# Weight splits ahead of the scatters, and the first expert block on two turns' rows

## The reference, cut to what matters

```python
def _moe_ref(x, w_gate, w_noise, noise, w1, w2):
    ...
    noisy_logits = logits + noise_scale * noise
    top2 = np.argpartition(-noisy_logits, 2, axis=1)[:, :2]
    ...
    for e in range(E):
        for k in range(2):
            mask = top2[:, k] == e
            h = np.maximum(x[mask] @ w1[e], 0.0)
            out[mask] += top2_w[mask, k, None] * (h @ w2[e])

def reference(**kwargs):
    attn_out = _attn_ref(...)            # 4 batches, 8 heads, 576 tokens, head size 64; pool = 8
    x = attn_out as (2304, 512)
    x = _moe_ref(x, ...)                 # E = 8, w1 (8, 512, 1024), w2 (8, 1024, 512)
    return _moe2_ref(x, ...)             # max(0.01 h, h) with h = x @ w_in (512, 2048), then @ w_out
```

## Time and profile before

| | |
|---|---|
| median of three runs | 1105.24 us |
| profiled execution | 1103.91 us |
| its span | 1102.2 us |
| PE busy | 1033.5 us (94%) |
| DVE busy | 378.9 us (34%) |
| POOL busy | 379.6 us (34%) |
| mean granted TensorE clock | 0.967 of 2.4 GHz |

### The profile page before, as it was taken

The page is one execution under the profiler, slowest core; times in us unless marked ns, Lnnn a source line. Parts: engine busy times, 40 slices in busy tenths (PEclk is TensorE's granted clock), DMA queues, the critical chain, the costliest instruction groups (busy, mean ns, idle before and its releaser), DMA issues.

```text
span 1102.2 us, 16369 instructions
## 1 busy us (share of the span) xinstructions
PE 1033.5 (94%) x5180; PEld 870.6 (79%) x5181; DVE 378.9 (34%) x678; ACT 272.5 (25%) x497; POOL 379.6 (34%) x413
## 2 busy tenths in 40 slices
PE   5988289999999999999999995899999999999998
PEld 4887268888888888888888884788888888888887
DVE  5988542122212221222122212653333333333222
ACT  3443012222222222222222220232222222222222
POOL 3338691280917355371908202950100100000000
PEclk9988589999999999999999997899999999999999
DMA  8945452151524333251514212421101101001000
GB/s 296 337 145 189 178 160 77 57 180 39 171 67 140 97 111 127 80 158 49 173 63 144 95 38 72 147 78 39 39 20 58 39 20 58 20 1 39 1 1 38
DMA packets 53779, 105.75 MB, mean 96 GB/s; under 512 B 7408, under 2 KB 7536, under 8 KB 53744
## 3 DMA queue, kind: packets, MB, share of 16 engines
q1 hardware_dynamic: 35312, 63.33, 18.1%
q10 hardware_dynamic: 12672, 23.07, 6.3%
q0 software_dynamic: 5760, 18.88, 5.1%
HBM read 77.47 MB, written 27.79 MB: 95 GB/s over the span
## 4 chain that ended last, share of the span: by engine, by line
PE 79%; issue 9%; DVE 7%; POOL 3%; DMA 1%; ACT 1%; SPq 0%; POOLq 0%; DVEq 0%; ACTq 0%
PE ps L603 23%; PE ps L605 23%; PE ps L604 23%; PE ps L629 3%; POOL w_split L467 2%; PE ps L561 2%; PE ps L610 1%; PE ps L539 1%; POOL w_split L465 1%; PE ps L671 1%; DVE maxima L906 1%; PE ps L549 1%; DVE x L1149 1%; DVE k_sum L892 1%; DMA k_raw<-in_kT_dram 1%
## 5 line engine op out<-in xcount | busy, mean ns | idle before, releaser
L467 POOL TENSOR_TENSOR w_split<-w_raw,w_split 128x512 fp32r<-128x512 f32 x144 | 186.3, 1294 | 12.0
L465 POOL TENSOR_SCALAR w_split<-w_raw 128x512 fp32r<-128x512 f32 x144 | 92.3, 641 | 226.7 <-PE ps L605 224.7
L603 PE MATMUL ps<-w_split,xs_hi 128*128 (+1 forms) x344 | 138.4, 402 | 3.9 <-DVE xs_lo L1108 3.9
L603 PE MATMUL ps<-w_split,hT_hi 128*128 (+1 forms) x344 | 139.0, 404 | 2.0 <-DVE hT_lo L1115 2.0
L605 PE MATMUL ps<-w_split,hT_lo 128*128 (+1 forms) x344 | 135.4, 394 | 0.0
L605 PE MATMUL ps<-w_split,xs_lo 128*128 (+1 forms) x344 | 134.7, 391 | 0.0
L604 PE MATMUL ps<-w_split,hT_hi 128*128 (+1 forms) x344 | 134.6, 391 | 0.0
L604 PE MATMUL ps<-w_split,xs_hi 128*128 (+1 forms) x344 | 134.6, 391 | 0.0
L492 POOL DMA_INDIRECT y_in<-y_blocks,y_rows x36 | 34.8, 968 | 269.1 <-DVE x L1149 194.8
L603 PE MATMUL ps<-x_hi,w_split 128*128 128x512 f32 (+1 forms) x320 | 120.5, 377 | 1.4 <-DVE x_lo L1157 1.4
L604 PE MATMUL ps<-x_lo,w_split 128*128 128x512 f32 (+1 forms) x320 | 118.8, 371 | 0.0
(11 more groups left out here) (147 smaller groups left out, 1505.3 us busy)
## 6 DMA issues: line engine op xcount, KB each, us to landing
w_raw<-in_wall_dram SPq DMA_DIRECT2D x160, 256.0 KB
xs<-x_sorted ACTq DMA_DIRECT2D x45, 256.0 KB, 2.7
y_blocks<-y_sb ACTq DMA_DIRECT2D x43, 256.0 KB, 2.0
k_raw<-in_kT_dram SPq DMA_DIRECT2D x16, 288.0 KB, 5.5
q_sb<-in_qT_dram SPq DMA_DIRECT2D x18, 256.0 KB, 5.2
v_raw<-in_vT_dram SPq DMA_DIRECT2D x16, 288.0 KB, 5.2
out_dram<-h_sb SPq DMA_DIRECT2D x10, 256.0 KB, 2.0
x_sorted<-zero_rows SPq DMA_DIRECT2D x9, 256.0 KB, 4.1
```

The costliest lines, as they stand in the source:

```text
L465: pool.tensor_scalar(hi, w_raw[:, a, :], 1.0, 0.0, ALU.mult, ALU.add).then_inc(split_hi, 1)
L467: pool.tensor_tensor(lo, w_raw[:, a, :], hi.bitcast(F32), ALU.subtract).then_inc(split, 1)
L603: pe.matmul(out_ap, lhs_hi, rhs_hi, start=first, stop=False)
```

## The change

- POOL does all 16 splits of expert 0 first, then the 36 scatters, turn by turn.
- SP's queue gets a new order: the nine zero writes stand later, in groups of four and five, chunks 8 to 15 earlier. SP waits for the scatters of turns 0 and 1 and tells ACT by `x_landed` = 1, then for the rest, and tells it by `x_landed` = 2.
- DVE writes `first_needs` after turn 1: 1 if expert 0 already has 128 rows or more, else 2. ACT reads it into a register and loads block 0 when `x_landed` has reached it.
- DVE does `split_rows(0)` before the lists, and `list_y_rows` after `split_h(1)` and no longer after `split_rows(0)`.
- PE takes block 0 whole before `up(1)`, with `turn_rows(1)` between the two halves of `down(0)`. Only after that it waits for the lists. ACT loads block 1 after `copy_h(0)`.
- Scratch tables of the lists move from `q_sb` to `probsT` and `probs`, out of the way of the block tiles.

```diff
@@ SP
-            sp.wait_ge(zeros_made, 1)
-            for row in ZEROED:
-                sp.dma_start(x_sorted[row:row + P, :], zero_rows[:, :]).then_inc(x_zeroed, 16)
             load_w(4)
...
             load_w(8)
+            load_v(13)
+            load_w(9)
             load_q(13)
-            load_v(13)
+            load_w(10)
             load_v(14)
-            load_w(9)
+            load_w(11)
+            sp.wait_ge(zeros_made, 1)
+            for row in ZEROED[0:4]:
+                sp.dma_start(x_sorted[row:row + P, :], zero_rows[:, :]).then_inc(x_zeroed, 16)
             load_q(14)
+            load_w(12)
             load_v(15)
-            load_w(10)
+            load_w(13)
+            for row in ZEROED[4:]:
+                sp.dma_start(x_sorted[row:row + P, :], zero_rows[:, :]).then_inc(x_zeroed, 16)
+            load_w(14)
+            load_w(15)
             load_q(15)
-            load_w(11)
             load_q(16)
             load_q(17)
-            for n in range(12, CHUNKS):
+            for n in range(CHUNKS, CHUNKS + RING):
                 load_w(n)
+            sp.wait_ge(x_sent_early, 16 * EARLY_SENT)
+            sp.sem_inc(x_landed, 1)
+            sp.wait_ge(x_sent_late, 16 * (2 * TILES - EARLY_SENT))
+            sp.sem_inc(x_landed, 1)
+            for n in range(CHUNKS + RING, 2 * CHUNKS):
+                load_w(n)
@@ POOL
-            for n in range(SPLIT_FIRST):
+            for n in range(CHUNKS):
                 split_chunk(n)
-            n = SPLIT_FIRST
             for turn in range(len(TURNS)):
-                rows = rows_of(turn)
-                for at in range(0, len(rows), 2):
-                    send_rows(turn, rows[at:at + 2])
-                    if n < CHUNKS:
-                        split_chunk(n)
-                        n += 1
+                send_rows(turn, rows_of(turn))
@@ PE
                 for k in range(KF):
+                    if first and k == KF // 2:
+                        turn_rows(b + 1)
                     if k % 4 == 0:
                         pe.wait_ge(hT_split, b * 2 + k // 4 + 1)
...
-            pe.wait_ge(lists_ready, 1)
             turn_rows(0)
             up(0, 0)
-            turn_rows(1)
             turn_h(0)
+            down(0, 0, True)
+            pe.wait_ge(lists_ready, 1)
             up(1, expert_of(1))
             turn_rows(2)
-            down(0, 0, True)
             turn_h(1)
@@ ACT
-            act.wait_ge(x_sent, 16 * 2 * TILES)
+            act.wait_ge(first_known, 1)
+            needed = act.value_load(first_needs[0:1, 0:1], min_val=1, max_val=2)
+            act.wait_ge(x_landed, needed)
             act.dma_start(xs[:, :], x_sorted[0:P, :]).then_inc(xs_in, 16)
+            copy_rows(0)
+            relu(0)
+            copy_h(0)
             act.wait_ge(lists_ready, 1)
-            copy_rows(0)
+            act.wait_ge(x_landed, 2)
             load_rows(1)
-            relu(0)
             copy_rows(1)
             load_rows(2)
-            copy_h(0)
@@ DVE
+                    if PLACE_AT.index(step) == EARLY_TURNS - 1:
+                        dve.tensor_scalar(first_needs[:, :], row_of[0:1, 0:1], float(P), 1.0, ALU.is_lt,
+                                          ALU.add).then_inc(first_known, 1)
...
+            split_rows(0)
             n_e, nb, end, start, val, last_row, first_moved, moved = (e8[:, j, :] for j in range(8))
...
-            split_rows(0)
+            split_h(0)
+            split_rows(1)
+            copy_y(0, True)
+            split_rows(2)
+            split_h(1)
             list_y_rows()
-            split_rows(1)
-            split_h(0)
-            split_rows(2)
-            copy_y(0, True)
-            split_h(1)
```

More of the change, by code:

```diff
@@ L52 @@
 ROWS = DUMMY + P
+EARLY_TURNS = 2
+EARLY_SENT = 2 * TURN_FROM[EARLY_TURNS]
 BLOCKS = (2 * TOKENS + EXPERTS * (P - 1)) // P
@@ L97, in build @@
         block_end = sb("block_end", [1, EXPERTS], I32)
-        sb("to_64_bytes", [1, EXPERTS])
+        first_needs = sb("first_needs", [1, 1], I32)
         sb("to_2048_bytes", [P, 120])
@@ L240, in build @@
         y_listed = sem("y_listed")
-        x_sent = sem("x_sent")
+        x_sent_early = sem("x_sent_early")
+        x_sent_late = sem("x_sent_late")
+        x_landed = sem("x_landed")
+        first_known = sem("first_known")
         x_zeroed = sem("x_zeroed")
@@ L361, in _ @@
             load_w(8)
+            load_v(13)
+            load_w(9)
             load_q(13)
-            load_v(13)
+            load_w(10)
             load_v(14)
-            load_w(9)
+            load_w(11)
+            sp.wait_ge(zeros_made, 1)
+            for row in ZEROED[0:4]:
+                sp.dma_start(x_sorted[row:row + P, :], zero_rows[:, :]).then_inc(x_zeroed, 16)
             load_q(14)
+            load_w(12)
             load_v(15)
-            load_w(10)
+            load_w(13)
[3 more added lines that the diff above has]
+            load_w(15)
             load_q(15)
-            load_w(11)
             load_q(16)
             load_q(17)
-            for n in range(12, CHUNKS):
+            for n in range(CHUNKS, CHUNKS + RING):
                 load_w(n)
-            with sp.Fori(1, STAGES) as s:
+            sp.wait_ge(x_sent_early, 16 * EARLY_SENT)
[4 more added lines that the diff above has]
+                load_w(n)
+            with sp.Fori(2, STAGES) as s:
                 for c in range(CHUNKS):
@@ L426, in send_rows @@
                         out_offset=bass.IndirectOffsetOnAxis(ap=slots_i[:, tile, k:k + 1], axis=0),
-                        in_=x_rows[:, tile, :], in_offset=None).then_inc(x_sent, 16)
+                        in_=x_rows[:, tile, :], in_offset=None).then_inc(
+                            x_sent_early if turn < EARLY_TURNS else x_sent_late, 16)
             def rows_of(turn):
@@ L472, in await_last_use @@
                 pool.wait_ge(blocks_done, end)
-            pool.wait_ge(x_sent, 16 * 2 * TILES)
+            pool.wait_ge(x_sent_early, 16 * EARLY_SENT)
+            pool.wait_ge(x_sent_late, 16 * (2 * TILES - EARLY_SENT))
             for c in range(CHUNKS):
@@ L1044, in _, with split_rows, split_h, copy_y @@
             then = link
+            def split_rows(b):
+                dve.wait_ge(xs_hi_made, b + 1)
+                dve.tensor_tensor(xs_lo[:, :, :].rearrange("p a b -> p (a b)"), ps[:, XT_BANK, :],
+                                  xs_hi[:, :, :].rearrange("p a b -> p (a b)").bitcast(F32),
+                                  ALU.subtract).then_inc(xs_split, 1)
+            def split_h(b):
+                for n in range(2):
+                    dve.wait_ge(hT_hi_made, b * 2 + n + 1)
+                    dve.tensor_tensor(hT_lo[:, 4 * n:4 * n + 4, :].rearrange("p a b -> p (a b)"),
+                                      ps[:, HT_BANK + n, :],
+                                      hT_hi[:, 4 * n:4 * n + 4, :].rearrange("p a b -> p (a b)").bitcast(F32),
+                                      ALU.subtract).then_inc(hT_split, 1)
+            def copy_y(b, first):
+                dve.wait_ge(blocks_done, b + 1)
+                if not first:
+                    dve.wait_ge(y_out, b * 16)
+                dve.tensor_copy(y_sb[:, :], ps[:, Y_BANK, :]).then_inc(y_copied, 1)
+            split_rows(0)
             n_e, nb, end, start, val, last_row, first_moved, moved = (e8[:, j, :] for j in range(8))
@@ L1103, in list_y_rows @@
                 weigh(len(TURNS) - 1)
[L1106 to L1114, removed]
-                    dve.tensor_tensor(hT_lo[:, 4 * n:4 * n + 4, :].rearrange("p a b -> p (a b)"),
-                                      ps[:, HT_BANK + n, :],
-                                      hT_hi[:, 4 * n:4 * n + 4, :].rearrange("p a b -> p (a b)").bitcast(F32),
-                                      ALU.subtract).then_inc(hT_split, 1)
-            def copy_y(b, first):
-                dve.wait_ge(blocks_done, b + 1)
-                if not first:
-                    dve.wait_ge(y_out, b * 16)
-                dve.tensor_copy(y_sb[:, :], ps[:, Y_BANK, :]).then_inc(y_copied, 1)
-            split_rows(0)
-            list_y_rows()
-            split_rows(1)
-            split_h(0)
-            split_rows(2)
-            copy_y(0, True)
-            split_h(1)
+            split_h(0)
[3 more added lines that the diff above has]
+            split_h(1)
+            list_y_rows()
             with dve.Fori(2, BLOCKS) as b:
```

10 lines of the change are left out of this document (5 added, 5 removed).

## The result

| set of runs | changed kernel | kernel before, same chip | ratio, 95% interval |
|---|---|---|---|
| first | 1112.37 us (1112.30 to 1114.11, 4 runs) | 1103.98 us | 1.0082 [1.0065, 1.0099] |
| E5 | 1094.56 us (1091.02 to 1096.62, 4 runs) | 1104.67 us | 0.9900 [0.9870, 0.9931] |
| E9 | 1091.91 us (1090.41 to 1095.06, 4 runs) | 1103.87 us | 0.9900 [0.9881, 0.9920] |
| E12 | 1110.32 us (1107.04 to 1114.08, 6 runs) | 1104.06 us | 1.0065 [1.0040, 1.0090] |

Measured against the forecast of 1091.0 (range 1085 to 1099), the change made the kernel slower: 1112.37. The same kernel, run again later, fell on both sides: slower in the first set and in E12, faster in E5 and E9. The kernel before stayed at 1104 in all of them. What differs is seen in the traces.

The account below looks back on a forecast made before the run. PE bounds the kernel, busy 94% of the span, so only the seam between routing and blocks could be gained. 14.3 - 0.6 + 0.5 = 14.2 us off the profiled 1103.91 gave 1089.7, so a 1091.0 median, range 1085 to 1099.

Parts of the forecast that it names:

- Turn 1's wait for DVE ends at 98 as before: POOL, turn 1's scatters: DVE's placing still ends their wait at 98.11, with turn 0's scatters done at 91.
- The 14 last scatters thus end where they did, 134.26: POOL, turns 2 and 3: turn 1 ends at 110.8, ahead of 116.80, so the last scatter's end stays at 134.26.
- 16th split at about 76, turn 0's run to 91: POOL: the 16th split ends at about 76 (bounds 72 to 83), turn 0's twelve scatters take 15.2 us.
- 7 us of slack cover the routing: POOL, between turn 0's scatters ending at 91 and DVE's mark at 98: 7 us to spare.
- Splits ahead, about 0: POOL: moving 8 splits, 16 us in all, ahead of the scatters neither gains nor loses time.
- DVE beside POOL, +0.5 (bounds -3 to +3): Small DVE operations slowed beside POOL's splits: about 3 us of excess mostly moves, 0.5 us gained.
- Block 0 earlier, 14.3: PE: block 0's transposes at 123.3 instead of 138.99, up(2) at 150.5 instead of 164.76, gaining 14.3 us.
- The wait for xs, forecast at 1.6: PE, middle of down(0): stands 1.6 us for block 1's rows, which follow the last scatter and land at 139.5.
- list_y_rows 0.6: DVE: the later list_y_rows delays split_rows(3), so up(3) starts at 163.4 instead of 162.8; 0.6 us lost, bounds 0 and 2.5.
- the low clock: Rival, chance 0.17: PE stays at 1.2 GHz through up(0) or longer, 1093.1 to 1103.7 us, mostly 1093 to 1099.
- the missing early start: Rival, chance 0.04: `first_needs` is 2 or x_landed comes late, so block 0 is not early: 1107.2 us.
- the held queue of SP: Rival, chance 0.06: chunks waiting for splits hold SP's queue; a 16th split after 88.7 delays all scatters, 1097.3 at 95.

Follow-up runs that it names:

- E5: The changed kernel itself run again, unaltered, in another group on one chip: 1094.56 us, ratio 0.9900.
- E9: The changed kernel itself run a third time, unaltered, in another group: 1091.91 us, ratio 0.9900.
- E12: The changed kernel itself run a fourth time, unaltered, in another group: 1110.32 us, ratio 1.0065.
- E14: Changed kernel's early block, but 8 splits, turn 0's scatters in one run, other 8 splits, then turns 1 to 3 in runs, SP's old order: 1110.86 us.
- E13: Changed kernel with POOL's and SP's old order (scatters between splits) and list_y_rows cut in two parts: 1096.23 us.
- E15: Changed kernel with a 0.64 us POOL filler operation after every two scatters of turns 0 and 1: 1098.35 us.
- E16: Changed kernel with POOL waiting before each pair of scatters until the pair before the last has landed, at most four in flight: 1105.38 us.
- E1: Kernel before with only the change's order of POOL's splits and scatters and of SP's queue, blocks as before: 1107.54 us, ratio 1.0035.
- E11: Changed kernel with chunks 8 to 15 of expert 0 split on only 64 of 512 columns: 1090.38 us.
- E2: Changed kernel with the early block kept but POOL's and SP's order of the kernel before: 1091.28 us, ratio 0.9884.

## Why the prediction was wrong

The step that failed: "Turn 1's wait for DVE ends at 98 as before", and with it "The 14 last scatters thus end where they did, 134.26". I asked what POOL's order does to POOL and to DVE, and not what an unbroken run of scatters does to PE's updates. By my own mark ("wrong if the last scatter moves by more than 3 us") it moved by 17.4.

- **16th split at about 76, turn 0's run to 91**: right (76.6, 91.9), SP's queue too.
- **7 us of slack cover the routing**: wrong in size. Turn 2 was placed 17.1 us later; the three pieces in the chain of waits that end at DVE sum to 10.24 + 1.53 + 5.56 = 17.3. A part of each is a wait that DVE would have had anyway: the updates that ended them came 9.65, 1.58 and 3.34 us late, 14.6 in all, and the other 2.5 us of the 17.1 are of the size seen without held updates. That the runs are the cause is shown by E14 against E13 in one group (with runs 1110.86, without 1096.23) and by E15, where pauses take the waits away beside E16, which kept them. Without held updates turn 2 is still 1.9 to 6.9 us late (118.65 in E9, 123.72 in E5).
- **Splits ahead, about 0, and DVE beside POOL, +0.5 (bounds -3 to +3)**: together a loss. E1, which holds both and had no update held, lost 3.9 us; how much of it is DVE's is not shown. By the Trainium skill, SBUF — State Buffer, section Who interferes with whom, a DVE instruction with two SBUF inputs contends with a GpSimd instruction that reads SBUF, so the crowded splits could be behind it. In E11's trace, with those splits cut to an eighth of their columns, the routing was no earlier (turn 1 at 104.22, E5 104.70), so this case does not bear that out as the cause.
- **Block 0 earlier, 14.3**: the mechanism was right (E2, with the old scatter order, gains 12.3 in all, what its lists cost already taken off). In the first set the transposes came at 140.78, not at 123.3, 17.5 late. Then relu(0) was held for 3.3 us. PE stood idle for it, and the granted clock fell to its lower level at 153.4, so that the first half of down(0) took 5.07 us (155.80 to 160.87) and not 2.72, which is 2.4 more. The wait for xs, forecast at 1.6, did not come and gives back a part: up(2) 21.2 late (171.65 against 150.5).
- **list_y_rows 0.6**: 1.5 in E2 and here (185.44 - 171.65 = 13.79), 0.9 more.
- Sum: 1089.7 + 21.2 + 0.9 = 1111.8 against the profiled 1112.3.
- **Rivals**: the low clock, apart from up(0) where it was forecast, showed for 4.4 us of down(0), as said above; the missing early start and the held queue of SP did not occur. The rival that happened was not on my list, though the chance of slower was put at 0.03.

E5 and E9 do not make the forecast right: there, the 1091.9 to 1094.6 include a last scatter that in the traces starts 2.1 and 7.2 us later than forecast (135.38 and 140.51 against 133.30). That E9's median is 0.9 from the forecast is in part luck.

What stays open: what it is in a set of runs that lets PE's updates be held. The kernel before has its profile in such a set (333 separate updates of 576) and loses nothing by it, since its scatters of turns 0 and 1 alternate with splits, and PE has next to nothing to do in its last run. The path on which the updates wait is not shown by any record. A rival that no run tests is the recording itself: every execution here was recorded by the profiler, the late updates come in just those groups whose traces lack records, and nothing shows how the kernel runs unrecorded.

## What to carry to other kernels

Where GpSimd issues many indirect DMAs in a row, TensorE's semaphore updates can come up to 10 us late, on some occasions and not on others; here work between them, even 0.6 us of filler after every two, kept them on time (E15, 80 to 125 us). So an interleaving that seems to serve only one engine's load may be what keeps the others going: ask of each unbroken run who has to signal during it. And a wait that ends with no releaser in the trace is to be checked against the end of the instruction that should have released it; if a result is far off, run the same kernel on another occasion before explaining it.

## What the hardware showed unexpectedly

- PE's updates were late by up to 10.18 us (E14) while POOL issued indirect DMAs 0.30 us apart, and came at the latest 2.5 us after the run's end. Those of DVE, ACT and POOL that the same traces record were on time (0.02 us).
- In those traces the scatters' 576 increments show as 107 to 334 updates, in the others as 564 to 576, and the last run shows it even in kernels whose earlier scatters alternate with other work (E15: 47 of 224). Records of DVE's updates are lacking there too.
- It follows the set of runs: four of seven sets had it, with the same program, on a chip of the same number, on either side (E9, E12).
